# Expert tiles of a two-layer mixture of experts: the W2 split ahead of the copy of the next rows, first rows turned from the ring, idle transposes paced by semaphores

## What is computed

```python
q_pool = q.reshape(B, H, S // 2, 2, D).mean(axis=3)      # B 4, H 8, S 1152, D 64
attn = softmax(scale * q_pool @ k.T);  x = attn @ v      # to 2304 x 512
...
# layer 1, for tokens with x @ w_skip > 0 (the others keep x)
e = argmax(x @ w_gate)
x = x + gate_w * (relu(x @ w1[e]) @ w2[e])
...
# layer 2, for all tokens
e = argmax(x @ w_gate);  eom = sigmoid(x @ w_output_gate)
out = gate_w * eom[e] * (relu(x @ w1[e]) @ w2[e])
```

## Time and profile before

| | us |
|---|---|
| median of 3 runs | 1163.72 (1163.67 to 1164.05) |
| the profiled execution | 1163.63, its span 1161.9 |
| TensorE matmuls busy | 1116.4 (96% of the span) |
| VectorE busy | 752.0 (65%) |
| ScalarE busy | 537.6 (46%) |
| GpSimd busy | 451.3 (39%) |
| mean granted TensorE clock | 0.981 of full |
| layer 1, from the first up matmul | 601.0 to 844.5 us of the span |
| layer 2 | from 847.2 to the end |

### The profile page before, as it was taken

One profiled execution on the slowest core, in us unless ns is written; L12 is line 12 of the kernel. 1 busy time (PEld: TensorE's weight loads), 2 busy tenths in 40 slices (PEclk: granted clock), 3 DMA queues, 4 the chain that ended last, 5 costly groups with the idle time before them and its releaser, 6 DMA issues.

```text
span 1161.9 us, 22128 instructions
## 1 busy us (share of the span) xinstructions
PE 1116.4 (96%) x7821; PEld 934.7 (80%) x7821; DVE 752.0 (65%) x1706; ACT 537.6 (46%) x945; POOL 451.3 (39%) x339
## 2 busy tenths in 40 slices
PE   7999999999999999999879999999789999999996
PEld 5777777777777777777678899988689999999995
DVE  7766668776687767886236777766645556655541
ACT  3556655555555555555323444343234534443320
POOL 0768876678666776668610000000100010000100
PEclk9999999999999999999978999999989999999999
DMA  5262225233222232222357414174592473141100
GB/s 127 65 224 72 62 73 144 62 86 99 62 73 72 76 100 73 62 52 58 134 176 272 148 36 182 42 303 157 194 331 92 170 260 111 37 172 36 45 10 14
DMA packets 74398, 132.61 MB, mean 114 GB/s; under 512 B 11040, under 2 KB 29472, under 8 KB 74320
## 3 DMA queue, kind: packets, MB, share of 16 engines
q1 hardware_dynamic: 43424, 50.58, 16.5%
q10 hardware_dynamic: 26240, 69.22, 16.3%
q0 software_dynamic: 4656, 11.79, 2.9%
HBM read 106.12 MB, written 19.24 MB: 108 GB/s over the span
## 4 chain that ended last, share of the span: by engine, by line
PE 82%; DVE 11%; issue 2%; DMA 2%; POOL 1%; SPq 0%; DVEq 0%; ACTq 0%; ACT 0%; POOLq 0%
PE PS L733 20%; PE PS L584 10%; PE PS L501 8%; PE PS L567 8%; PE PS L554 7%; PE PS L750 6%; PE PS L746 6%; PE PS L568 6%; PE PS L747 6%; DVE mx L1036 3%; PE PS L621 1%; DVE W2L L1144 1%; PE PS L765 1%; PE PS L612 1%; PE PS L597 1%
## 5 line engine op out<-in xcount | busy, mean ns | idle before, releaser
L443 POOL TENSOR_TENSOR arena_a<-arena_a,arena_p 128x576 f32<-128x576 f32 x224 | 331.0, 1478 | 99.3 <-ACT arena_p L849 81.2
L1036 DVE TENSOR_REDUCE mx<-PS 128x1 f32<-128x384 f32 (+1 forms) x480 | 246.3, 550 | 111.6 <-PE PS L554 108.5
L733 PE MATMUL PS<-moe,W 128*128 128x128 f32 x2432 | 281.5, 277 | 1.5 <-ACT moe L935 1.5
L733 PEld LDWEIGHTS PS<-moe,W 128*128 128x128 f32 x2432 | 278.6, 193 | 3.9 <-ACT moe L935 2.1
L849 ACT ACTIVATE arena_p<-PS 128x576 f32<-128x576 f32 x288 | 187.3, 651 | 153.4 <-PE PS L568 141.3
L567 PE MATMUL PS<-QHT,KA 128*128 128x288 f32 x576 | 191.8, 337 | 0.5 <-ACT QLT L860 0.5
L554 PE MATMUL PS<-KA,QHT 128*128 128x384 f32 (+1 forms) x480 | 174.0, 363 | 5.5 <-DVE mx L1036 4.9
L568 PE MATMUL PS<-QLT,KB 65*128 65x288 f32 x576 | 169.0, 297 | 0.0
L821 ACT CAST W2H<-W2R 128x1024 fp32r<-128x1024 f32 x148 | 144.2, 1048 | 51.5 <-PE PS L750 41.0
L1144 DVE TENSOR_TENSOR W2L<-W2R,W2H 128x1024 fp32r<-128x1024 f32 x144 | 166.4, 1217 | 0.0
L584 PE MATMUL PS<-arena_p,arena_a 128*64 128x288 f32 x1152 | 160.5, 414 | 0.0
(11 more groups left out here) (174 smaller groups left out, 1185.9 us busy)
## 6 DMA issues: line engine op xcount, KB each, us to landing
W<-in_moe_w ACTq DMA_DIRECT2D x16, 2048.0 KB, 14.3
W2R<-in_moe_w ACTq DMA_DIRECT2D x16, 2048.0 KB, 9.1
moe<-xs SPq DMA_DIRECT2D x40, 258.0 KB, 2.7
arena_a<-in_k SPq DMA_DIRECT2D x32, 288.0 KB, 3.0
arena_a<-in_v SPq DMA_DIRECT2D x32, 288.0 KB, 2.8
KB<-KA SPq DMA_DIRECT2D x32, 288.0 KB, 3.1
arena_a<-in_q SPq DMA_DIRECT2D x32, 256.0 KB, 3.2
xs<-padrow SPq DMA_DIRECT2D x8, 258.0 KB, 3.4
```

Source lines behind the costliest of these rows:

```text
L443: nc.gpsimd.tensor_tensor(Acc[u], Acc[u], P[u][:, t, :], ALU.add).then_inc(acc_step, 1)
L733: last = nc.tensor.matmul(PS[:, HB + f // 4, (f % 4) * PN:(f % 4 + 1) * PN], W1[s][:, d, f * PN:(f + 1) * PN], xT[:, d, :], start=(d == 0) ...
L1036: vec.reduce_max(mx3[0:n, t, c:c + 1], PS[0:n, MXB + b % 2, 0:KB_], AX.X).then_inc(pr_max, 1)
```

## The change

1. In VectorE's tile loop `w2_low` stands ahead of the ring slot's load and the copy to `xa`.
2. The first tile's transposes (`trans_first`) read the ring itself and wait for `x_in` alone. SP waits for them before it loads over slot 0.
3. SP writes one pad less (expert 5), ScalarE's queue one more.
4. TensorE's idle transposes: before layer 1, 50 + 24 become 28, six times 9 behind a wait for `handed`, and 18; Pool raises `handed` behind each of its last six scatters. Before layer 2, 20 (then the wait for the first rows) and 4 become 30, a wait for `tables[1]`, 12, a wait for `ob_free`, and 22.

```diff
--- before.py
+++ after.py
@@ -310,7 +310,7 @@
         t_chain = sem("t_chain")
         cnt_mm = sem("cnt_mm")
         ob_free = sem("ob_free")
-        sent = sem("sent")
+        sent, handed = sem("sent"), sem("handed")
         def pad_regions(eng, m, experts):
 
             eng.wait_ge(counts[m], 1)
@@ -390,7 +390,7 @@
                     sp.wait_ge(ob_free, 1)
                 sp.wait_ge(pad_first[m], 16)
                 sp.dma_start(xring[:, 0:ROW], xs[ds(first, PN), :]).then_inc(x_in[m], 16)
-                pad_regions(sp, m, range(E // 2 + 1, E))
+                pad_regions(sp, m, range(E // 2 + 2, E))
 
                 def load_x(i, slot):
                     row = sp.value_load(row_i[m][0:1, ds(i, 1)], min_val=0, max_val=NR * RS - PN)
@@ -400,6 +400,7 @@
                 for n in range(1, XR):
                     sp.wait_ge(x_in[m], 16 * n)
                     load_x(n, n)
+                sp.wait_ge(xt_done[m], 1)
                 with sp.Fori(0, tiles - (XR - 1)) as i:
                     slot = sp.value_load(ring_i[0:1, ds(i, 1)], min_val=0, max_val=XR - 1)
                     sp.wait_ge(xa_done[m], i + 1)
@@ -465,7 +466,9 @@
                     first_w2_low(SPLIT_IN.index(h))
                 if h in SCATTER_IN:
                     scatter_rows(*SCATTER_IN[h])
-            scatter_rows(B - 1)
+            for t in range(TB):
+                scatter_rows(B - 1, [t])
+                pool.sem_inc(handed, 1)
 
 
             def scatter_tile(i):
@@ -713,16 +716,26 @@
             pe.wait_ge(wr_in, 32)
             pe.wait_ge(rt_acc, B)
             nc.tensor.matmul(PS[0:1, 5, 0:NR], onesb[:, 0:1], Raccb[:, :], start=True, stop=True).then_inc(cnt_mm, 1)
-            keep_busy(50, TR)
+            keep_busy(28, TR)
+            for t in range(TB):
+                pe.wait_ge(handed, t + 1)
+                keep_busy(9, TR)
             for u in range(2):
                 pe.wait_ge(rt_scat[u], 16 * TB * (B // 2))
-            keep_busy(24, TR)
+            keep_busy(18, TR)
 
             def trans_x(m, i):
 
                 pe.wait_ge(xa_done[m], i + 1)
                 for d in range(DC):
                     last = transpose(PS[:, XTB, d * PN:(d + 1) * PN], xa[:, d * PN:(d + 1) * PN])
+                last.then_inc(xt_done[m], 1)
+
+            def trans_first(m):
+
+                pe.wait_ge(x_in[m], 16)
+                for d in range(DC):
+                    last = transpose(PS[:, XTB, d * PN:(d + 1) * PN], xring[:, d * PN:(d + 1) * PN])
                 last.then_inc(xt_done[m], 1)
 
             def up(m, i, s):
@@ -773,7 +786,7 @@
 
             for m in range(2):
                 pe.wait_ge(tables[m], 1)
-                trans_x(m, 0)
+                trans_first(m)
                 start = 0
                 for e in range(E):
                     w = m * E + e
@@ -801,9 +814,11 @@
                     keep_busy(8, TR)
                     pe.wait_ge(rt_acc, start + (B + 1))
                     nc.tensor.matmul(PS[0:1, LB, 0:NR], onesb[:, 0:1], Raccb[:, :], start=True, stop=True).then_inc(cnt_mm, 1)
-                    keep_busy(20, TR)
-                    pe.wait_ge(x_in[1], 16)
-                    keep_busy(4, TR)
+                    keep_busy(30, TR)
+                    pe.wait_ge(tables[1], 1)
+                    keep_busy(12, TR)
+                    pe.wait_ge(ob_free, 1)
+                    keep_busy(22, TR)
 
 
         @block.scalar
@@ -929,7 +944,7 @@
                 if m == 0:
                     for u in range(2):
                         act.wait_ge(rt_scat[u], 16 * TB * (B // 2))
-                pad_regions(act, m, range(1, E // 2 + 1))
+                pad_regions(act, m, range(1, E // 2 + 2))
                 act.wait_ge(tables[m], 1)
                 act.wait_ge(xt_done[m], 1)
                 nc.scalar.copy(xT, PS[:, XTB, 0:DM].rearrange("p (c n) -> p c n", c=DC)).then_inc(xt_out[m], 1)
@@ -1284,13 +1299,13 @@
                     w = m * E + e
                     end = dve.value_load(tend_i[m][0:1, e:e + 1], min_val=e + 1, max_val=MAXT)
                     with dve.Fori(start, end) as i:
+                        if w + 1 < 2 * E:
+                            w2_low(m, w + 1, i * WCH + (WCH if m == 0 else 0))
                         slot = dve.value_load(ring_i[0:1, ds(i + 1, 1)], min_val=0, max_val=XR - 1)
                         dve.wait_ge(x_in[m], i * 16 + 32)
                         dve.wait_ge(xt_done[m], i + 1)
                         dve.wait_ge(xk_done[m], i + 1)
                         vec.tensor_copy(xa, xring[:, ds(slot * ROW, ROW)]).then_inc(xa_done[m], 1)
-                        if w + 1 < 2 * E:
-                            w2_low(m, w + 1, i * WCH + (WCH if m == 0 else 0))
                         h_low(m, i, 0)
                         h_low(m, i, 1)
                         if m == 0:
```

## The result

| | before | after |
|---|---|---|
| median | 1163.81 us (1163.67 to 1164.05, 4 runs) | 1175.01 us (1172.46 to 1176.32, 4 runs) |
| the profiled execution | 1163.63, span 1161.9 | 1176.09, span 1174.3 |
| mean granted TensorE clock | 0.981 | 0.986 |

The account below looks back on a forecast made before the run. TensorE holds 82% of the chain, so changes elsewhere count only where it waits. The terms 14.4 - 1.5 + 2.0 + 1.1 - 5.5 + 1.6 + 1.6 - 4.6 + 0.2 give +9.3 us: 1173 us, range 1166 to 1184.

Parts of the forecast that it names:

- Subtractions ahead of the copy: Layer one's 14 later tiles: the late copy makes TensorE wait, +14.4 us; old waits at L750 go, -1.5.
- The old waits' -1.5: Layer one's later tiles: waits at L750 for the hi/lo remainder go, -1.5 us, bounds 0 and 2.7.
- the second tile's extras: Layer one, tile 1: +2.0 us from ScalarE's queue holding the high parts, and +1.6 for a clock fall.
- The rule of the sum: Layer one's tiles: TensorE doesn't wait if the copy ends within 7.22 us of the up matmuls' start.
- Tile 1 behind ScalarE's queue: Layer one, tile 1: third weight load delays ScalarE's high parts; 3.3 us wait instead of 1.3, +2.0 us.
- Layer one's start: Layer one, tile 0: fifth pad delays the evacuation, +1.1 us; no wait at L750, -5.5; clock fall, +1.6.
- The -5.5: Layer one, tile 0: L750 doesn't wait, so the tile takes 14.6 us, not 20.1.
- The clock: Layer one: TensorE's clock falls behind the long waits of tiles 0 and 1, +1.6 us each.
- the rival of a fall in every new-expert tile: Layer one: waits of 1.26 us drop the clock, six more falls at 1.6, +9.6, 1183 us; chance 0.13.
- Layer two (-4.6): Layer two, first tile: up matmuls 1.5 us sooner at full clock, 0.8 of waiting, -4.6 us, bounds -1.0 and -5.4.
- Ring load hidden: VectorE's loop: the ring's register load is hidden behind the subtractions; rival that it isn't: +14, 1187 us, chance 0.05.
- 13.07 us for layer two's other tiles: Layer two after its first tile: tiles unchanged at 13.07 us, +0.2 us in all.

Follow-up runs that it names:

- e3_two_ahead: The changed kernel with two of the four subtractions ahead of the copy and two behind it: 1162.17 us, 0.9991 of before.
- e2_order_only: The kernel before with VectorE's new order (four subtractions ahead of the copy) and nothing else: 1173.71 us, 1.0096 of before.
- e4_three_ahead: The changed kernel with three subtractions ahead of the copy and one behind it: 1163.23 us, 0.9993 of before.
- e5_two_ahead_pads_back: The changed kernel with two subtractions ahead of the copy and the fifth pad back on SP's queue: 1160.52 us, 0.9967 of before.
- e1_copy_first: The changed kernel with the old order on VectorE, copy ahead of the four subtractions: 1166.45 us, 1.0026 of before.
- e8_two_ahead_pads_early_split: The changed kernel with two subtractions ahead of the copy and SP's two layer-two pads issued before the `ob_free` wait: 1162.36 us, 0.9995 of before.
- e9_two_ahead_weights_early: The changed kernel with two subtractions ahead of the copy and ScalarE's two layer-two weight loads issued behind layer one's last tile: 1158.41 us, 0.9947.

## Why the prediction was right, and where it was off

The forecast was 1173 us, slower; the median is 1175.0. Step by step:

- **Subtractions ahead of the copy (+14.4 - 1.5).** Right in mechanism and nearly in size. Forecast were 1.26 us of waiting at a new expert and 0.67 within one. Tiles now take 15.76 and about 15.2 to 15.3 where 14.60 is the time without any wait (e3_two_ahead), so 1.16 and some 0.6 to 0.7 longer; of this TensorE's idle time is 0.97 and about 0.5, and the rest shows in no wait. Ahead of the first subtraction VectorE idled 0.56 us at a new expert, waiting for ScalarE's cast, and not at all within one; the sum had 0.7 and 0.1. The old waits' -1.5 is what e3_two_ahead shows. Tiles 1 to 13 were forecast at +15.3 with the second tile's extras (14.4 - 1.5 = 12.9, less tile 14's 1.2, is 11.7; + 2.0 + 1.6); they measured 5.55 + 9.03 = +14.6.
- **Threshold.** The rule of the sum, that the copy must end within 7.22 us of the up matmuls' start, held: three ahead ends it at 7.16 and is free, four ahead is not.
- **Tile 1 behind ScalarE's queue (+2.0, clock +1.6).** Right. The changed kernel, ScalarE's queue, its casts, VectorE and TensorE:

```profile
618.38 4.32 ACTq L827 DMA_DIRECT2D W<-in_moe_w  x1
623.49 3.89 ACT L836 CAST W2H<-W2R 128x1024 fp32r<-128x1024 f32 x4 [6.07 <-issue]
```

```profile
624.57 4.63 DVE L1159 TENSOR_TENSOR W2L<-W2R,W2H 128x1024 fp32r<-128x1024 f32 x4 [3.38 <-ACT W2H L836]
```

```profile
618.41 7.39 PE L746 MATMUL PS<-moe,W 128*128 128x128 f32 x64
629.60 1.58 PE L504 MATMUL PS<-ident,moe 128*128 128x128 f32 x8 [3.79 <-DVE moe L1308]
```

  The wait is 3.79 us where 3.3 was forecast.
- **Layer one's start (+1.1 - 5.5 + 1.6 = -2.8).** Right: +1.35 and -3.84, together -2.5. Five pads held ScalarE's queue for 5.43 us, and TensorE stood 3.25:

```profile
595.99 5.43 ACTq L319 DMA_DIRECT2D xs<-padrow  x5
...
602.16 3.06 PE L746 MATMUL PS<-moe,W 128*128 128x128 f32 x15 [3.25 <-ACT moe L950]
```

  The -5.5 doesn't need this edit: e2_order_only has it from the order alone, at 14.80 us. Added to that order the edit costs. The `handed` waits paced nothing, as forecast: Pool's sequencer had raised all six by 589.2, while the last of its six scatters started at 592.25, and the last 34 idle transposes ran without a break.

```profile
L471 POOLq EVENT_SEMAPHORE  x6: 17/17/17, 585.7 to 589.2; - x6
```

```profile
594.54 3.93 PE L504 MATMUL PS<-ident 128*128 128x128 f32 x34 [0.15 <-issue]
```

- **The clock (+1.6 in tile 0, +1.6 in tile 1).** Both falls came. In the tiles of the changed kernel the clock fell beside the three long waits and not beside the short ones; windows of its profile (length, busy and count of five engines, granted clock, DMA share, GB/s):

```profile
602.10:609.40 7.30, 7.24 (x50) 7.24 (x51) 5.66 (x6) 4.49 (x6) 0.00 (x0) 0.77 0.24 67
629.60:634.00 4.40, 4.40 (x17) 3.75 (x18) 1.14 (x2) 1.17 (x2) 0.00 (x0) 0.61 1.04 413
640.00:840.00 200.00, 190.99 (x1366) 173.02 (x1366) 133.61 (x398) 86.21 (x143) 14.74 (x13) 1.00 0.41 149
859.10:866.50 7.40, 7.35 (x64) 7.22 (x64) 4.63 (x4) 4.38 (x5) 0.00 (x0) 1.00 0.93 266
869.00:876.60 7.60, 7.56 (x29) 6.29 (x30) 1.18 (x2) 0.59 (x1) 0.00 (x0) 0.78 1.04 398
```

  It was at 0.77, 0.61 and 0.78 behind gaps of 3.25, 3.79 and 2.48 us, and was 1.00 from 640 to 840 us, through all the waits of tiles 2 to 14. That refutes the rival of a fall in every new-expert tile. But the sum let the length of the wait decide, and across the runs it doesn't. Ahead of tile 0's up matmuls, e4_three_ahead stood longer than e5_two_ahead_pads_back and kept its clock; the row and its window, first e4_three_ahead, then e5_two_ahead_pads_back:

```profile
602.75 7.41 PE L746 MATMUL PS<-moe,W 128*128 128x128 f32 x64 [3.06 <-ACT moe L950]
602.70:610.00 7.30, 7.25 (x64) 7.25 (x65) 4.53 (x5) 4.40 (x6) 0.00 (x0) 1.00 0.22 66
```

```profile
604.10 9.04 PE L746 MATMUL PS<-moe,W 128*128 128x128 f32 x64 [2.09 <-ACT moe L950]
604.10:611.40 7.30, 7.30 (x50) 7.30 (x51) 2.36 (x2) 4.48 (x5) 0.00 (x0) 0.77 0.39 116
```

  It was 1.00 as well behind 2.95 us in e1_copy_first and 2.87 in e8_two_ahead_pads_early_split. So that tile 0's fall came in this profiled execution was luck, as far as these runs show. Its price wasn't: tile 0 took 16.25 us with the fall, and 14.60 without it in e4_three_ahead and e8_two_ahead_pads_early_split, which have the same edits at layer one's start: 1.65, where I had 1.6. In tile 1 the time beyond 14.60 and the wait of 3.79 is 1.8.

  The Trainium skill (TensorE: Matmul & The Clock Gate, What's actually happening) has the clock fall only after a whole idle spell of its own counting; as I read it, 2.48 us would have been let off. The trace doesn't agree (0.78 behind it), as it didn't before (0.53 behind 2.05 us).
- **Layer two (-4.6): the step that failed.** I added up that the up matmuls start at full clock, 1.5 us sooner, and that the second rows land 8.1 us after the first weight load's issue, for a wait of 0.8. The full clock came (1.00 from 859.1), but only 1.0 us of the 1.5: the up matmuls started 9.6 us behind the start of Pool's last scatter (849.53), and before 10.6 (836.54). The second rows were copied at 868.56, 10.0 us behind the load's issue at 858.53. TensorE waited 2.48 us, and the clock fell in the same tile. I had taken the 8.1 us from before's one tile as if the rows' time hung on that issue alone. It hangs on a chain of three: two pads, their landing, then the rows, the last two beside 4 MB of weights; e9_two_ahead_weights_early, without these, shows 2.8 us for the rows and no wait. Tile 14 with its way to layer two and this first tile came out at +0.6 us together; the forecast had -4.6 + 1.2 (tile 14's own wait) = -3.4. This 4.0 us is more than the whole miss of the span, 12.5 against 9.3; the other terms came out 0.8 lower. The forecast had named a gain of only 1 us here as part of its range, for a clock that falls and rows as late as before; with tile 14's own wait taken off, it was 0.6.
- **Ring load hidden, 13.07 us for layer two's other tiles:** both as forecast. The copy starts right behind the fourth subtraction, and the last row of the table by stretches is unchanged.

## What to carry to other kernels

Where an engine works in program order, count for each piece of work when the next engine needs it, and put ahead of it only as much as its slack holds: here, with two subtractions ahead, 1.2 us of slack were left; the third cost nothing, and the fourth 10 us in twelve tiles. What fills an idle stretch pays only if the stretch behind it has its inputs; look next at the small transfers, and start large ones where they don't run beside a small one that something waits for.

## What the hardware showed that I had not expected

- A load of 258 KB took 6.8 and 6.9 us from issue to use beside two loads of 2 MB (the changed kernel, e3_two_ahead), and 2.8 without them (e9_two_ahead_weights_early).
- A semaphore raised by GpSimd behind its indirect DMAs doesn't pace its reader by those DMAs: all six were raised by 589.2 us, and the sixth DMA started at 592.25.
- The granted clock behind a wait doesn't follow from the wait's length: 1.00 behind 2.87, 2.95 and 3.06 us, but 0.77 behind 2.09. What else decides is open.
- The changed kernels vary more from run to run than before's first runs did: 3.9 us between the lowest and highest of four runs of after, 4.6 in ten of e1_copy_first. Before itself spread from 1161.9 to 1168.2 over 25 runs. In the profiled runs what differs at equal code is the stretch to attention's end (584.3 to 587.8 us) and whether tile 0 saw a fall of the clock. What sets the first is open too; no run isolates it.
